# The high and low parts of w_a and w_b: taken apart by pieces in the attention stage instead of during the expert search

## The chip, the cores and the metric

One core of one Trainium2 chip. The metric is the device time of one execution in microseconds (us). Engines are named as in the profile: PE is TensorE (PEld its weight loads), DVE is VectorE, ACT is ScalarE, POOL is GpSimd, SP is SyncE; a "q" behind a name is that engine's queue, from which transfers are issued. The profile gives PE's granted clock as a share of 2.4 GHz: 1.00 is 2.4 GHz and 0.50 is 1.2 GHz.

## The reference, cut to what matters

```python
# attention: B, H, S, D = 4, 8, 768, 40
for t in range(S):
    m_new = maximum(f[t] + m, i[t])
    C = exp(f[t] + m - m_new) * C + exp(i[t] - m_new) * outer(v[t], k[t])
    n = exp(f[t] + m - m_new) * n + exp(i[t] - m_new) * k[t]
    y[t] = sigmoid(o[t]) * (C @ q[t]) / maximum(abs(n @ q[t]), 1)
# experts: 3072 tokens of 320, 8 experts, 384 tokens to each
logits = x @ w_gate
# the highest logits first: a token goes to an expert that has room
out[mask] = relu(x[mask] @ w1[e]) @ w2[e]          # F = 1024
# third layer, for every token
a = x @ w_a;  b = x @ w_b;  out = (a * b) @ w_out   # 320 -> 1536 -> 320
```

Everything is float32. The kernel multiplies in a shorter format (fp32r) and keeps the precision by splitting each matrix in two: the high part is the matrix rounded to fp32r, the low part is the matrix less its high part.

## The kernel before, in words

**Attention** (`attention`, from L85). The sequence is cut in C = 6 chunks of 128 steps; with B = 4 batches that makes 24 units, u = 4c + b. Each engine walks through the units in its own order, and they are tied by semaphores. The first and the last chunk are written out; the four between run in a hardware loop (`each`, L47).

- PE, per unit: psI from the state (L444), psC from wv (L452), the logits of unit u-2 (L418), psO (L461, after DVE's prob), then the scores psS of unit u+1 (L404), the exponents psE of unit u+2 (L395) and the transposes psT of unit u-1 (L412).
- ACT, per unit: the exponential of psE (L356), the issue of three transfers of q (L329), in the unit with b = 3 also the sigmoid of the gates with two table loads (L322, L363), then the store of y of unit u-2 (L343) and the copy xt of the transposes of unit u-2 (L348), for which it waits.
- POOL, per unit: st_old from the state (L286), wv of the next unit (L258), the mask of the next unit (L264, on the tile decay), and the new state (L271), for which it waits for DVE's L592.
- DVE, per unit: prob (L581), the normalization of the unit before (L559), num from psI (L586), the gated y of the unit before (L570), st_add from psC (L592; the profile calls its tile work), the logits' copy (L553), then, waiting for psO, **the sum of the values** num + psO (L598), denh (L600), den (L602) and the reciprocal (L605), on which the next normalization depends.
- SP issues the loads of qks and toks some four units ahead, after the scores and the psO of the unit whose buffers are refilled, and once a chunk the rows and the gates.

After its last unit POOL writes the whole numbers that the search needs into `ints` (L294 to L303).

**Search and experts** (`experts`, from L674). DVE and PE search for the first expert to be full in 11 rounds: DVE compares (cmp, L1133), PE counts (psT, L967 and L978), DVE narrows the range (L1191, with eq and key at L1195 and L1197 after some rounds). Then DVE picks the tokens (L1204 on) and places them (at_slot, L1270), POOL gathers them (L852), and PE starts on w1 and w2 of the first expert. The eight turns of the experts follow, each with the third layer (L929 to L952), which reads w_a and w_b as wa and wb: [128, 5, 1536], blocks 0 and 1 the high parts of rows 0 to 255, block 2 the high part of rows 256 to 319 in partitions 0 to 63 and its low part in partitions 64 to 127, blocks 3 and 4 the low parts of rows 0 to 255.

wa and wb are filled at the start of `experts`, beside the search: SP loads both matrices whole (L831 to L834), ACT copies the high parts (L1074 to L1076, two instructions of 128 x 4608), and POOL subtracts: L858, two instructions of 64 x 1536, and L863, eight of 128 x 768. POOL's gather (L852) stands behind them.

Of the kernel before, what the change touches and what calls it, by code (L numbers as in the profile page):

```python
# [16 lines left out]
P = 128  # L17
# [37 lines left out]
def build(nc, qk, tok, ig, fg, w_gate, w1, w2, w_a, w_b, w_out, out, xs, parts):  # L55
    with ExitStack() as ctx:
        logit = ctx.enter_context(nc.sbuf_tensor("logit", [P, TILES, E], F32))
        identf = ctx.enter_context(nc.sbuf_tensor("identf", [P, P], F32))

        wa = ctx.enter_context(nc.sbuf_tensor("wa", [P, 5, F2], F32R))  # L60
        wb = ctx.enter_context(nc.sbuf_tensor("wb", [P, 5, F2], F32R))
        second = (wa, wb)
        fixed = search_tensors(nc, ctx)
        with ExitStack() as inner:
            attention(nc, inner, logit, identf, qk, tok, ig, fg, w_gate, xs, parts, fixed)
        with ExitStack() as inner:
            experts(nc, inner, logit, identf, second, w_a, w_b, w_out, w1, w2, xs, out, fixed)
# [17 lines left out]
def attention(nc, ctx, logit, identf, qk, tok, ig, fg, w_gate, xs, parts, fixed):  # L85
# [53 lines left out]
    ints = sb("ints", [P, 384], I32)  # L139
# [21 lines left out]
    y_out1 y_out0 row_in parts_out diag_done st_scaled masked mrow_zero made cast_done reloaded""".split()  # L161
# [5 lines left out]
    block = ctx.enter_context(nc.Block())  # L167

# [4 lines left out]
    def _(sp):  # L173
# [3 lines left out]
        def load_gates(c):  # L177
            sp.dma_start(gate[:, bass.ds(c, 1), :, :].rearrange("p c b n -> p (c b) n"),
                         tok[bass.ds(c, 1), :, :, TOK:TOK + DM].rearrange("c b t n -> t (c b) n")).then_inc(sm["og_in"], 16)

# [9 lines left out]
        def chunk(c):  # L190
            for b in range(B):
# [20 lines left out]
                else:  # L212
                    sp.wait_ge(sm["o_ready"], u - B + 1)
                    sp.dma_start(toks[b][:, 0:TOK], tok[bass.ds(c, 1), b, :, 0:TOK].rearrange("c t n -> (c t) n")).then_inc(tok_in[b], 16)
                    if b == 1:
                        sp.wait_ge(sm["e_ready"], c * B)
                        load_rows(c)
            if not (isinstance(c, int) and c == C - 1):
                load_gates(c + 1)
        each(sp, C, chunk)  # L220

    @block.gpsimd
    def _(pool):
# [56 lines left out]
        for u in range(TILES):  # L280
# [12 lines left out]
            new_state(u)  # L293
        pool.iota(rowi, [[P, C], [S, B]], base=0, channel_multiplier=1).then_inc(sm["made"], 1)  # L294
# [18 lines left out]
    def _(act):  # L313
# [5 lines left out]
        def open_gates(c):  # L319
            act.wait_ge(sm["og_in"], 16 * (c + 1))  # L320
            g = gate[:, bass.ds(c, 1), :, :].rearrange("p c b n -> p (c b n)")
            act.activation(g, g, ACT.Sigmoid).then_inc(sm["gate_ready"], 1)  # L322

# [26 lines left out]
        def chunk(c):  # L350
            for b in range(B):
# [6 lines left out]
                if not (isinstance(c, int) and c == C - 1 and b):  # L358
                    load_turned(u + B - 1, (c + 1, b - 1) if b else (c, B - 1))
                if b == 3 and not (isinstance(c, int) and c == C - 1):  # L360
# [115 lines left out]
    def _(dve):  # L476
# [95 lines left out]

        def chunk(c):
            for b in range(B):
# [18 lines left out]
                if not (isinstance(c, int) and c == 0 and b < 2):  # L593
                    keep_logits(u - 2, (c, b - 2) if b > 1 else (c - 1, b + 2))

# [78 lines left out]
def experts(nc, ctx, logit, identf, second, w_a, w_b, w_out, w1, w2, xs, out, fixed):  # L674
# [24 lines left out]
    wab_in = ("wa_in", "wb_in")  # L699
# [5 lines left out]
    a_sb = [sb(f"a_sb{n}", [P, CAP]) for n in range(2)]  # L705
    ab = [sb(f"ab{n}", [P, CAP]) for n in range(2)]
# [15 lines left out]
    h_lo = [sb(f"h_lo{n}", [P, CAP], F32R) for n in range(2)]  # L722
    ab_hi = [sb(f"ab_hi{n}", [P, CAP], F32R) for n in range(2)]
# [74 lines left out]
    wa_in wb_in wab_hi wab_lo member_ready ranked x2_mm out_mm slots_ready slots_mm expert_known grouped parts_ready""".split()  # L798
# [17 lines left out]
    def _(sp):  # L816
# [30 lines left out]
    def _(pool):  # L847
# [31 lines left out]
    def _(pe):  # L879
# [49 lines left out]
        def pair(k, g, between_a=None, between_b=None):  # L929
            if isinstance(k, int) and k == 0 and g % GQ == 0:  # L930
                pe.wait_ge(sm["wab_lo"], 2 + 2 * (g // GQ + 1))
# [121 lines left out]
    def _(act):  # L1053
# [14 lines left out]
        def high_out(q):  # L1068
            act.wait_ge(wo_in[q % 2], 16 * (q // 2 + 1))
            if q == 0:  # L1070
                act.wait_ge(sm["wab_lo"], 2 + 2 * Q)
# [9 lines left out]
        def turn(k, beside):  # L1081
# [23 lines left out]
            for g in range(GT):  # L1105
                act.wait_ge(sm["ab_mm"], k * GT + g + 1)
                at_least(act, sm["ab_done"], k * GT + g - 1)
                if early and g == 0:
                    act.wait_ge(sm["wab_lo"], 2 + 2 * Q)
# [368 lines left out]
```

## Time and profile before

| | us |
|---|---|
| median of 3 runs | 939.88 (936.88 to 940.74) |
| the profiled execution | 947.86 |
| its span, first to last instruction | 946.1 |
| PE busy | 820.5 (87%) |
| DVE busy | 619.5 (65%) |
| ACT busy | 273.4 (29%) |
| POOL busy | 169.3 (18%) |
| attention | to about 163 |
| search, until PE starts on w1 | about 163 to 226 |
| eight turns of the experts | about 226 to 946 |

The profiled execution took 947.86 us, 1.7 us more than its span. Times in rows are counted from the start of the span. A row of the timeline has the start, the duration, engine, line, operation, the tile written and the tiles read, their shapes and the count; what stands in brackets is how long the engine had been idle before it and who ended that. Matmul rows of one group are merged.

### The profile page before, as it was taken

The page shows a single profiled execution, that of the slowest core. Times are in us where ns is not written, and L with a number is a line of the kernel's source. Part 1 is how long each engine was busy: PE and PEld are TensorE (multiplying, and loading weights), DVE is VectorE, ACT ScalarE, POOL GpSimd, SP SyncE. Part 2 cuts the span into 40 slices and gives each one's busy share as a digit, 9 for nine tenths or more (in the row PEclk, how much of TensorE's full clock was granted, in tenths as well). Part 3 has the DMA queues.
Part 4 walks back from the last instruction along what each step waited for, and adds up shares of the span by engine and source line. Part 5 has one row for each costly group of instructions (what it writes and reads, how often), then busy time and mean ns, then how long its engine had stood idle before and what let it go on. Part 6 is the DMA issues. An engine that isn't in the chain of part 4 may idle for free.

```text
span 946.1 us, 16640 instructions
## 1 busy us (share of the span) xinstructions
PE 820.5 (87%) x5858; PEld 757.7 (80%) x5858; DVE 619.5 (65%) x1644; ACT 273.4 (29%) x490; POOL 169.3 (18%) x195
## 2 busy tenths in 40 slices
PE   1999997314799899979997999899989989999995
PEld 1999997214689878978897889789878988998995
DVE  7688888576557865785677557755876683374222
ACT  4444441302223412331233123312422241233221
POOL 6665664261000110000011001100110011011001
PEclk9999999555789999999998999999999999999998
DMA  4766651612202200220031004100400120041000
GB/s 118 242 211 214 218 171 48 186 28 85 73 21 82 84 21 1 69 76 21 0 99 65 0 0 115 48 0 11 132 21 0 61 82 21 1 131 35 1 1 21
DMA packets 51620, 66.60 MB, mean 70 GB/s; under 512 B 6376, under 2 KB 42232, under 8 KB 51576
## 3 DMA queue, kind: packets, MB, share of 16 engines
q1 hardware_dynamic: 37352, 50.31, 17.5%
q0 software_dynamic: 2368, 7.88, 2.9%
q10 hardware_dynamic: 11856, 7.87, 2.7%
q8 instruction: 22, 0.36, 0.1%
q14 instruction: 22, 0.18, 0.1%
HBM read 57.88 MB, written 8.16 MB: 70 GB/s over the span
## 4 chain that ended last, share of the span: by engine, by line
PE 48%; DVE 23%; issue 5%; ACT 4%; DMA 2%; POOL 1%; ACTq 0%; DVEq 0%; POOLq 0%
PE psA L897 18%; PE acc L920 11%; PE psB L897 8%; PE acc L947 6%; DVE at_slot L1270 2%; DVE ab L1356 2%; DVE w_lo L1294 2%; DMA xg<-xs_dram,idx_g 2%; DVE cmp L1133 2%; ACT ab_hi L1103 2%; DVE w_lo L1290 2%; DVE ab_lo L1360 1%; DVE w_hi L1292 1%; PE psT L978 1%; DVE o_sb L1437 1%
## 5 line engine op out<-in xcount | busy, mean ns | idle before, releaser
L897 PE MATMUL psA<-x_hi,wa 128*128 128x384 f32 x480 | 136.1, 348 | 0.5 <-DVE x_lo L1382 0.4
L897 PE MATMUL psB<-x_hi,wb 128*128 128x384 f32 x480 | 131.8, 339 | 0.0
L852 POOL DMA_INDIRECT xg<-xs_dram,idx_g x24 | 24.9, 1036 | 466.8 <-DVE idx_g L1284 462.0
L1110 ACT COPY a_sb<-psA 128x384 f32<-128x384 f32 x96 | 46.1, 481 | 193.0 <-PE psB L897 193.0
L897 PE MATMUL psA<-x_lo,wa 128*128 128x384 f32 x288 | 96.8, 336 | 0.0
L897 PE MATMUL psB<-x_lo,wb 128*128 128x384 f32 x288 | 96.5, 335 | 0.0
L947 PE MATMUL acc<-wo_hi,ab_hi 128*128 128x320 f32 x288 | 92.1, 320 | 1.0 <-DVE ab_lo L1360 1.0
L1089 ACT ACTIVATE h_hi<-psA 128x384 fp32r<-128x384 f32 x64 | 31.5, 492 | 205.9 <-PE psA L897 197.9
L1356 DVE TENSOR_TENSOR ab<-a_sb,psB 128x384 f32<-128x384 f32 x96 | 53.0, 552 | 55.6 <-ACT a_sb L1110 55.2
L947 PE MATMUL acc<-wo_lo,ab_hi 128*128 128x320 f32 x288 | 88.8, 308 | 0.0
L947 PE MATMUL acc<-wo_hi,ab_lo 128*128 128x320 f32 x288 | 88.7, 308 | 0.0
L897 PE MATMUL psA<-x_hi,w_hi 128*128 128x384 f32 x192 | 76.5, 399 | 13.5 <-DVE w_lo L1297 7.5
L1360 DVE TENSOR_TENSOR ab_lo<-ab,ab_hi 128x384 fp32r<-128x384 f32 x96 | 53.6, 559 | 52.2 <-ACT ab_hi L1103 48.2
L897 PEld LDWEIGHTS psA<-x_hi,wa 128*128 128x128 f32 x480 | 83.1, 188 | 4.1 <-DVE x_lo L1382 2.1
L897 PEld LDWEIGHTS psB<-x_hi,wb 128*128 128x128 f32 x480 | 86.0, 188 | 0.1
L920 PE MATMUL acc<-h_hi,w_hi 128*128 128x384 f32 x192 | 73.0, 380 | 14.5 <-DVE h_lo L1349 14.5
L1103 ACT CAST ab_hi<-ab 128x384 fp32r<-128x384 f32 x96 | 49.2, 513 | 82.7 <-DVE ab L1356 80.3
L897 PE MATMUL psA<-x_lo,w_hi 128*128 128x384 f32 x192 | 67.9, 354 | 0.0
L920 PE MATMUL acc<-h_lo,w_hi 128*128 128x384 f32 x192 | 67.3, 350 | 0.0
L920 PE MATMUL acc<-h_hi,w_lo 128*128 128x384 f32 x192 | 67.2, 350 | 0.0
L874 POOL DMA_INDIRECT out_dram<-o_sb,idx_s x24 | 23.7, 986 | 219.9 <-DVE o_sb L1437 215.0
L947 PEld LDWEIGHTS acc<-wo_hi,ab_hi 128*128 128x128 f32 x288 | 54.1, 188 | 2.1 <-DVE ab_lo L1360 1.2
(236 smaller groups left out, 1744.7 us busy)
## 6 DMA issues: line engine op xcount, KB each, us to landing
w_raw<-in_w_dram SPq DMA_DIRECT2D x32, 320.0 KB, 3.3
w_raw<-in_w_dram SPq DMA_DIRECT2D x32, 256.0 KB, 3.0
toks<-in_tok_dram SPq DMA_DIRECT2D x24, 324.0 KB, 3.5
qks<-in_qk_dram SPq DMA_DIRECT2D x48, 160.0 KB
w_raw<-in_w_dram SPq DMA_DIRECT2D x64, 64.0 KB, 2.8
gate<-in_tok_dram SPq DMA_DIRECT2D x6, 640.0 KB, 5.4
xs_dram<-y ACTq DMA_DIRECT2D x24, 160.0 KB, 3.2
qst<-in_qk_dram ACTq DMA_DIRECT2D x48, 60.0 KB
```

Of the source, the lines that this page charges most:

```text
L852: pool.indirect_dma_start(out=xg[:, t, 0:DM], out_offset=None, in_=xrows, in_offset=bass.IndirectOffsetOnAxis(ap=idx_g[:, t:t + 1], axis=0 ...
L874: pool.indirect_dma_start(out=out, out_offset=bass.IndirectOffsetOnAxis(ap=idx_s[:, t:t + 1], axis=0), in_=o_sb[:, t, :], in_offset=None). ...
L897: last = pe.matmul(ps, w, x, start=(n == 0), stop=(n == len(steps) - 1))
L920: last = pe.matmul(acc[m][:, 0:CAP], w[q][:, f % FQ, c], x[n][:, :], start=(f == 0 and j == 0), stop=(f == FT - 1 and j == 2))
L947: last = pe.matmul(acc[t][:, 0:DM], x[n][:, c], w[:, g, :], start=(g == 0 and j == 0), stop=(g == GT - 1 and j == 2))
L1089: act.activation(h_hi[f % 2][:, :], psA[f % 2][:, 0:CAP], ACT.Relu).then_inc(sm["h_hi_ready"], 1)
L1103: act.copy(ab_hi[g % 2][:, :], ab[g % 2][:, :]).then_inc(sm["ab_hi_ready"], 1)
L1110: act.copy(a_sb[g % 2][:, :], psA[g % 2][:, 0:CAP]).then_inc(sm["a_copied"], 1)
L1133: dve.scalar_tensor_tensor(out=cmp[:, :, :], in0=key[lv][:, :].unsqueeze(2).broadcast_to([P, TILES, 16]), scalar=start_at[:, lv:lv + 1] if ...
L1270: dve.tensor_tensor(at_slot[i][:, :, :], prow[:, i * ST:(i + 1) * ST].unsqueeze(2).broadcast_to([P, ST, P]), slot[:, :].unsqueeze(1).broad ...
L1356: dve.tensor_tensor(ab[g % 2][:, :], a_sb[g % 2][:, :], psB[g % 2][:, 0:CAP], ALU.mult).then_inc(sm["ab_done"], 1)
L1360: dve.tensor_tensor(ab_lo[g % 2][:, :], ab[g % 2][:, :], f32(ab_hi[g % 2][:, :]), ALU.subtract).then_inc(sm["ab_ready"], 1)
```

## The change

SP, in the attention stage, loads w_a and w_b in six pieces of 256 columns each (`load_piece`, three transfers, 384 KB together), two units or more ahead of their use. ACT copies the high part of a piece of w_a in the units with b = 0 and of a piece of w_b in those with b = 2, behind its exponential and its issues (`split_high`, 128 x 768). DVE subtracts half a piece in every unit, between the logits' copy and the sum of the values (`split_low`): two instructions, 128 x 256 and 64 x 128 (partitions 64 to 127). `ints` now lies in the piece's buffer, so POOL waits for the last subtraction before it writes there. In `experts` the loads, the two copies, POOL's ten subtractions and the waits for them are gone.

```diff
+    piece = sb("piece", [P, 2, 3, F2 // C])
+    ints = piece[:, 0, :, :].rearrange("p k f -> p (k f)").bitcast(I32)
+    FB = F2 // C
...
+        def load_piece(c, i):
+            at_least(sp, sm[f"piece_lo{i}"], 4 * c)
+            w, cols = (w_a, w_b)[i], bass.ds(c * FB, FB)
+            sp.dma_start(piece[:, i, 0:2, :], w[0:2 * P, cols].rearrange("(k p) f -> p k f", p=P)).then_inc(sm[f"piece_in{i}"], 16)
+            sp.dma_start(piece[0:64, i, 2, :], w[2 * P:DM, cols]).then_inc(sm[f"piece_in{i}"], 16)
+            sp.dma_start(piece[64:P, i, 2, :], w[2 * P:DM, cols]).then_inc(sm[f"piece_in{i}"], 16)
...
                     if b == 1:
                         sp.wait_ge(sm["e_ready"], c * B)
                         load_rows(c)
+                    if b == 0:
+                        load_piece(c - 1, 1)
+                if b == 2:
+                    load_piece(c, 0)
...
         each(sp, C, chunk)
+        load_piece(C - 1, 1)
...
             new_state(u)
+        for i in range(2):
+            pool.wait_ge(sm[f"piece_lo{i}"], 4 * C)
...
+        def split_high(c, i):
+            act.wait_ge(sm[f"piece_in{i}"], 48 * (c + 1))
+            act.copy(second[i][:, 0:3, bass.ds(c * FB, FB)], piece[:, i, :, :]).then_inc(sm[f"piece_hi{i}"], 1)
...
                     load_turned(u + B - 1, (c + 1, b - 1) if b else (c, B - 1))
+                if b % 2 == 0:
+                    split_high(c, b // 2)
...
+        def split_low(c, b):
+            i = b // 2
+            w, at = second[i], b % 2 * (FB // 2)
+            part, cols = slice(at, at + FB // 2), bass.ds(c * FB + at, FB // 2)
+            dve.wait_ge(sm[f"piece_hi{i}"], c + 1)
+            dve.tensor_tensor(w[:, 3:5, cols], piece[:, i, 0:2, part], w[:, 0:2, cols].bitcast(F32), ALU.subtract).then_inc(sm[f"piece_lo{i}"], 1)
+            dve.tensor_tensor(w[64:P, 2, cols], piece[64:P, i, 2, part], w[64:P, 2, cols].bitcast(F32), ALU.subtract).then_inc(sm[f"piece_lo{i}"], 1)
...
                     keep_logits(u - 2, (c, b - 2) if b > 1 else (c - 1, b + 2))
+                split_low(c, b)
 
                 dve.wait_ge(sm["o_ready"], u + 1)
...
-    with nc.sbuf_tensor("wab_raw", [P, 2, 3, F2], F32) as wab_raw:
-        pass
...
-        for i, w in enumerate((w_a, w_b)):
-            sp.dma_start(wab_raw[:, i, 0:2, :], w[0:2 * P, :].rearrange("(k p) f -> p k f", p=P)).then_inc(sm[wab_in[i]], 16)
-            sp.dma_start(wab_raw[0:64, i, 2, :], w[2 * P:DM, :]).then_inc(sm[wab_in[i]], 16)
-            sp.dma_start(wab_raw[64:P, i, 2, :], w[2 * P:DM, :]).then_inc(sm[wab_in[i]], 16)
...
-        for i in range(2):
-            pool.wait_ge(sm["wab_hi"], i + 1)
-            pool.tensor_tensor(second[i][64:P, 2, :], wab_raw[64:P, i, 2, :], f32(second[i][64:P, 2, :]), ALU.subtract).then_inc(sm["wab_lo"], 1)
-        pool.wait_ge(sm["wab_lo"], 2)
-        for q in range(Q):
-            cols_ = slice(q * GQ * P, (q + 1) * GQ * P)
-            for i in range(2):
-                pool.tensor_tensor(second[i][:, 3:5, cols_], wab_raw[:, i, 0:2, cols_], f32(second[i][:, 0:2, cols_]), ALU.subtract
-                                   ).then_inc(sm["wab_lo"], 1)
-        pool.wait_ge(sm["wab_lo"], 2 + 2 * Q)
...
-        for i in range(2):
-            act.wait_ge(sm[wab_in[i]], 48)
-            act.copy(second[i][:, 0:3, :], wab_raw[:, i, :, :]).then_inc(sm["wab_hi"], 1)
```

The buffers a_sb and ab are declared further down, with the same sizes.

## Rows read from the trace of the kernel before

**Rows 1.** Stretches view: length, busy us and count by engine, clock, DMA share, GB/s.

```profile
20.00:163.00 143.00, 140.01 (x1478) 133.53 (x1478) 120.32 (x268) 53.73 (x69) 84.14 (x107) 1.00 0.59 184
```

**Rows 2.** Timeline, PE: the second and the last score products.

```profile
31.30 1.16 PE L404 MATMUL psS<-qks 40*128 40x128 f32 x16
...
152.57 1.16 PE L404 MATMUL psS<-qks 40*128 40x128 f32 x16
```

**Rows 3.** Timeline, DVE: one unit and the next one's start.

```profile
126.58 1.23 DVE L581 TENSOR_TENSOR prob<-psS,decay 128x1024 f32<-128x1024 f32 x1
...
128.53 1.06 DVE L570 TENSOR_TENSOR y<-work,gate 128x320 f32<-128x320 f32 x1
129.51 0.49 DVE L592 TENSOR_TENSOR work<-psC,diag 120x328 f32<-120x328 f32 x1
...
130.41 0.50 DVE L598 TENSOR_TENSOR num<-num,psO 128x328 f32<-128x328 f32 x1 [0.34 <-PE psO L461]
130.95 0.17 DVE L600 TENSOR_SCALAR denh<-num 128x8 f32<-128x8 f32 x1
131.15 0.61 DVE L602 SCALAR_TENSOR_TENSOR den<-num,denh 128x8 f32<-128x8 f32 x1
...
131.99 1.22 DVE L581 TENSOR_TENSOR prob<-psS,decay 128x1024 f32<-128x1024 f32 x1
...
133.94 0.48 DVE L570 TENSOR_TENSOR y<-work,gate 128x320 f32<-128x320 f32 x1
```

**Rows 4.** Timeline, POOL: the same unit.

```profile
128.16 1.09 POOL L264 TENSOR_SCALAR_AFFINE_SELECT decay<-decay 128x1024 f32<-128x1024 f32 x1 [1.13 <-ACT decay L356]
130.15 0.89 POOL L271 TENSOR_TENSOR state<-st_old,work 120x328 f32<-120x328 f32 x1 [0.90 <-DVE work L592]
130.99 0.74 POOL L286 TENSOR_TENSOR st_old<-state,dec 120x328 f32<-120x328 f32 x1
131.68 0.74 POOL L258 TENSOR_TENSOR wv<-toks,gw 128x328 f32<-128x328 f32 x1
```

**Rows 5.** Waits view, 60 to 150 us (us in total, times, longest).

```profile
ACT xt L348 <- PE psT L412: 51.6, 13, 4.1
```

**Rows 6.** Chain of waits, search stage (start us, us, what).

```profile
169.09 0.63 DVE cmp L1133
...
175.66 0.26 DVE eq L1195
...
178.41 3.77 DVE cmp L1133
...
188.12 1.76 DVE eq L1195
...
195.45 2.27 DVE cmp L1133
...
203.12 1.89 DVE sel L1204
```

**Rows 7.** Timeline, POOL: the first low part.

```profile
178.34 3.42 POOL L858 TENSOR_TENSOR wa<-wab_raw,wa 64x1536 fp32r<-64x1536 f32 x1 [18.52 <-ACT wa L1076]
```

**Rows 8.** Timeline, ACT and DVE: the same operations on other weights.

```profile
213.55 0.83 ACT L1064 CAST w_hi<-w_raw 128x768 fp32r<-128x768 f32 x1 [27.62 <-DMA w_raw<-in_w_dram]
...
215.98 0.42 DVE L1292 TENSOR_TENSOR w_hi<-w_raw,w_hi 64x256 fp32r<-64x256 f32 x1
...
217.29 0.29 DVE L1297 TENSOR_TENSOR w_lo<-w_raw,w_hi 128x128 fp32r<-128x128 f32 x1
```

**Rows 9.** Timeline, ACT, SP and DVE: the first units.

```profile
25.72 1.02 ACT L356 ACTIVATE decay<-psE 128x1024 f32<-128x1024 f32 x1 [1.22 <-PE psE L395]
...
25.91 0.48 SPq L211 DMA_DIRECT2D toks<-in_tok_dram  x1
...
32.58 1.23 DVE L581 TENSOR_TENSOR prob<-psS,decay 128x1024 f32<-128x1024 f32 x1
```

**Rows 10.** DMA issues of the attention stage (KB each, median us to landing).

```profile
toks<-in_tok_dram SPq DMA_DIRECT2D x22, 324.0 KB, 3.5
```

More of the change, by code:

```diff
@@ L64, in build @@
         with ExitStack() as inner:
-            attention(nc, inner, logit, identf, qk, tok, ig, fg, w_gate, xs, parts, fixed)
+            attention(nc, inner, logit, identf, second, w_a, w_b, qk, tok, ig, fg, w_gate, xs, parts, fixed)
         with ExitStack() as inner:
-            experts(nc, inner, logit, identf, second, w_a, w_b, w_out, w1, w2, xs, out, fixed)
+            experts(nc, inner, logit, identf, second, w_out, w1, w2, xs, out, fixed)
 def search_tensors(nc, ctx):
@@ L82, in search_tensors, with attention @@
     }
-def attention(nc, ctx, logit, identf, qk, tok, ig, fg, w_gate, xs, parts, fixed):
+def attention(nc, ctx, logit, identf, second, w_a, w_b, qk, tok, ig, fg, w_gate, xs, parts, fixed):
     def sb(name, shape, dt=F32):
@@ L137, in attention @@
     scaled = work[0][:, 0:DM]
-    ints = sb("ints", [P, 384], I32)
+    piece = sb("piece", [P, 2, 3, F2 // C])
+    ints = piece[:, 0, :, :].rearrange("p k f -> p (k f)").bitcast(I32)
     rowi, tilei, pi, digiti = ints[:, 0:24], ints[:, 24:48], ints[:, 48:49], ints[:, 64:80]
@@ L160, in attention @@
     state_done i_used o_used den_half den_done r_done scale_done y_ready og_in gate_ready wv_ready wg_zero y_zero
-    y_out1 y_out0 row_in parts_out diag_done st_scaled masked mrow_zero made cast_done reloaded""".split()
+    y_out1 y_out0 row_in parts_out piece_in0 piece_in1 piece_hi0 piece_hi1 piece_lo0 piece_lo1 diag_done st_scaled masked mrow_zero made cast_done reloaded""".split()
     sm = {n: sem(n) for n in names}
@@ L671, with experts @@
 GI = GJ * 16
-def experts(nc, ctx, logit, identf, second, w_a, w_b, w_out, w1, w2, xs, out, fixed):
+def experts(nc, ctx, logit, identf, second, w_out, w1, w2, xs, out, fixed):
     def sb(name, shape, dt=F32):
@@ L698, in experts @@
     wa, wb = second
-    wab_in = ("wa_in", "wb_in")
-    with nc.sbuf_tensor("wab_raw", [P, 2, 3, F2], F32) as wab_raw:
-        pass
     wo_hi = sb("wo_hi", [P, GT, DM], F32R)
     wo_lo = sb("wo_lo", [P, GT, DM], F32R)
-    a_sb = [sb(f"a_sb{n}", [P, CAP]) for n in range(2)]
-    ab = [sb(f"ab{n}", [P, CAP]) for n in range(2)]
     w1_raw = [sb(f"w1_raw{n}", [P, 3, FQ * P]) for n in range(2)]
@@ L722, in experts @@
     h_lo = [sb(f"h_lo{n}", [P, CAP], F32R) for n in range(2)]
+    a_sb = [sb(f"a_sb{n}", [P, CAP]) for n in range(2)]
+    ab = [sb(f"ab{n}", [P, CAP]) for n in range(2)]
     ab_hi = [sb(f"ab_hi{n}", [P, CAP], F32R) for n in range(2)]
@@ L797, in experts @@
     wo_hi_done wo_split made counted spread given_ready given_sum v_step cmp_ready full_ready
-    wa_in wb_in wab_hi wab_lo member_ready ranked x2_mm out_mm slots_ready slots_mm expert_known grouped parts_ready""".split()
+    member_ready ranked x2_mm out_mm slots_ready slots_mm expert_known grouped parts_ready""".split()
     sm = {n: sem(n) for n in names}
@@ L929, in pair @@
         def pair(k, g, between_a=None, between_b=None):
-            if isinstance(k, int) and k == 0 and g % GQ == 0:
-                pe.wait_ge(sm["wab_lo"], 2 + 2 * (g // GQ + 1))
             at_least(pe, sm["ab_done"], k * GT + g - 1)
@@ L1069, in high_out @@
             act.wait_ge(wo_in[q % 2], 16 * (q // 2 + 1))
-            if q == 0:
-                act.wait_ge(sm["wab_lo"], 2 + 2 * Q)
             act.copy(wo_hi[:, q * GQ:(q + 1) * GQ, :], wo_raw[q % 2]).then_inc(sm["wo_hi_done"], 1)
-        for i in range(2):
-            act.wait_ge(sm[wab_in[i]], 48)
-            act.copy(second[i][:, 0:3, :], wab_raw[:, i, :, :]).then_inc(sm["wab_hi"], 1)
         high_parts(0, 0)
@@ L1107, in turn @@
                 at_least(act, sm["ab_done"], k * GT + g - 1)
-                if early and g == 0:
-                    act.wait_ge(sm["wab_lo"], 2 + 2 * Q)
                 act.copy(a_sb[g % 2][:, :], psA[g % 2][:, 0:CAP]).then_inc(sm["a_copied"], 1)
```

## The prediction, made before the changed kernel ran

> **What bounds the kernel now.** I read the stretches first, then the timelines of PE, DVE and POOL over one unit, the waits, and last the chain of waits through the search. In attention PE is busy 140 of 143 us at the full clock [rows 1]: it runs without a gap, and its score products start at 31.30 for unit 1 and 152.57 for unit 23 [rows 2], so a unit takes 121.27 / 22 = 5.51 us. DVE is close behind. The unit shown goes from prob at 126.58 to prob at 131.99, 5.41 us, and DVE idles only 0.34 of it, in front of the sum of the values [rows 3]. DVE is also held up by POOL. The gated y takes 1.06 us while POOL's mask runs and 0.48 one unit later without it; it ends 0.34 after the mask, the time of its 320 columns. den has 8 columns, takes 0.61, and ends 0.03 after POOL's st_old [rows 3, 4]. So a DVE instruction with two SBUF inputs waits out a POOL instruction. The sum of the values and prob, which read PSUM, keep their 0.50 and 1.22. In the search the same happens with longer partners: cmp takes 0.63, but 3.77 beside POOL's low part of 3.42, which began just before it [rows 6, 7]. These cmp lie on the chain.
>
> **What goes: the search.** Seven DVE instructions are stretched by POOL's ten subtractions: cmp 3.77; eq 1.76 and its like behind it, key, 1.85; three cmp of 2.11, 2.27 and 2.27; sel 1.89. Together 15.92. Undisturbed they are four cmp of 0.63, two of 0.26 as eq, and sel about 0.17 as denh in rows 3: 3.21. Gain 12.7 us, all on the chain [rows 3, 6]. ACT's two copies, the six loads and POOL's waits there are covered by the search and give nothing more: the gather waits for the token list anyway.
>
> **What comes: DVE.** The 128 x 256 instruction costs what 64 x 256 does, 0.42, the 64 x 128 one what 128 x 128 does, 0.29 [rows 8]. Both have two SBUF inputs, and they stand just where POOL starts its three instructions state, st_old, wv. So I lay the unit out from the end of st_add, 130.00 (129.51 + 0.49), with a waiting instruction taken in turn:
> - State first (it starts 0.15 after st_add; the logits' copy and the loop's address work may delay DVE that long). State ends 131.04, the first subtraction 0.28 later (256 columns against 320 in 0.34), 131.32. st_old takes 0.69 (spacing 130.99 to 131.68), to 132.01; the second subtraction, 132.15; wv 0.70, 132.85. The sum of the values runs 132.18 to 132.68, denh then waits for wv, 132.88, and den (0.20 with its gap), reciprocal (0.23) bring prob to 133.31. It was 131.99: 3.31 us after st_add, not 1.99.
> - Subtraction first: it ends 130.49, state about 131.30, the second subtraction 131.44, st_old 132.14, wv 132.84, den 132.87, prob 133.10: 3.10 after st_add.
>
> On the other side of the unit, the mask comes earlier against DVE, as it is timed by PE through the exponential. y then goes back from 1.06 to 0.48 and the normalization, which ends 1.6 after prob, is held by some 0.12: prob to the end of st_add goes from 3.42 to 2.96. The unit becomes 6.06 to 6.27, middle 6.17, against PE's 5.51. Between the two orders I take the middle, since neither row decides a difference of some hundredths. 22 units x 0.66 = 14.5 us. PE's work of a unit still fits: it has idle time in front of psO instead.
>
> By the Trainium skill ("SBUF — State Buffer", section "Who interferes with whom") VectorE and GpSimd share an exclusive lock: a VectorE instruction with two SBUF inputs and a GpSimd instruction that reads SBUF block one another in full, in order of issue. It speaks against this change, and its order of issue would give 3.10 or 3.31 as above; the stretched y, den and cmp agree with it, while without such a lock the sum is that of the first rival.
>
> **ACT and SP.** The high part is 0.83 for 128 x 768 [rows 8], in every second unit, where ACT waits about 4 us in front of xt [rows 5]: nothing, if the piece has arrived. Piece 0 of a chunk is issued two units before its copy is due in DVE, but ACT comes to it right behind an early exponential. With three issues of about 0.5 each and 3.5 us to landing as for toks [rows 9, 10], it lands 5 us after the psO that releases the load, and the copy ends about when xt becomes ready. If that cover is gone, xt, the logits and the next exponential move. I take 1 us for all chunk borders, bounds 0 and 5. SP's own queue has room: about 2.5 us of issues in a unit of 5.5, and qks behind the piece moves by 1.5 us, more than a unit ahead of need. POOL's wait at the end finds the subtractions done; the last unit's fall into an idle stretch of DVE.
>
> **The start.** The first piece can't be ahead. SP issues it behind toks of 25.91, so from 26.4 to about 28, and it lands near 31.5 [rows 9, 10]. ACT copies to 32.4, and only then comes the exponential that ran at 25.72; its mask adds 1.1, and prob of unit 1 starts at about 34.6 rather than 32.58: 2.0 us. Bounds 0.5 (landing at 30) and 4 (a crowded start).
>
> **The sum.** -12.7 + 14.5 + 1.0 + 2.0 = +4.8 us. Against the profiled execution of 947.9 that is 952.7; the median of the runs shown is 8 us lower, and as the terms are differences within one execution I put them on that median: 939.9 + 4.8 = 944.7. A difference of 0.5%, 4.7 us, is about what a measurement of this kernel can tell from no change.
>
> **The rivals.**
> 1. Faster: the subtractions cost DVE only their own time. In place they take about 0.75 us (0.42 + 0.29, and starts that no longer overlap); a unit without DVE's wait is 5.41 - 0.34 = 5.07, so 5.82 against 5.51, 0.31 x 22 = 6.8. With 3.0 for start and borders: 939.9 - 12.7 + 9.8 = 937.0. If y is no longer held up, PE stays the bound and it is 930.2. It decides if the unit stays below 5.51 + 9.7 / 22 = 5.95. For it: in many units y loses half a microsecond to the mask that it could win back. Against: den would have to get in front of wv, and it comes 0.7 us too late. Centre 934.
> 2. POOL never yields: both subtractions wait for all three of its instructions. They end at 132.97 and prob comes at 134.13, a unit of 7.1: 22 x 1.6 = 35, 965. Against: denh at 130.95 runs in 0.17 between state and st_old [rows 3, 4].
> 3. The pieces come late in each chunk, 2 us for each of five, on top of the main case: 954. For it: twelve pieces of 384 KB add 4.6 MB to some 26 MB (184 GB/s for 143 us), with the DMA share at 0.59 already [rows 1].
> 4. The search's stretches are not POOL's doing, so nothing is gained: 957. Rows 6 and 7 speak plainly against it.
>
> TensorE: the stage before runs at 2.4 GHz with PE busy throughout [rows 1]. The gaps of 0.7 us that I expect in each unit leave it busy nine tenths of the time, and I cost them at nothing more.
>
> **Chances.** The main case 0.52; its own range is 22 units of 0.44 to 0.86, start 0.5 to 4 and borders 0 to 5, mostly 938 to 953. Rival 1 0.28, rival 2 0.05, rival 3 0.12, rival 4 0.03. Faster than 935.2: 0.20 of rival 1 and 0.04 of the main case, 0.24. Within: 0.08 and 0.20, 0.28. Slower than 944.6: 0.28 and the other three, 0.48. The range 931 to 956 leaves out rivals 2 and 4 and the tail of rival 1, and takes in rival 3.
>
> **What would show it.** In the changed profile the cmp of the search are all 0.63, and from the first cmp to at_slot it is 12 to 13 us shorter. The psS of units 1 and 23 are 135 to 137 us apart, not 121; PE idles in front of psO, waiting for prob; the two subtractions take 0.4 to 1.3 us with POOL's state or st_old ending just before them, and den ends just after wv. prob of unit 1 starts at 34 to 35. ACT's xt has an idle time in front of it in the units with b = 0. The prediction is wrong if psS keeps a distance below 5.95 a unit, or if the experts' turns, which nothing here touches, change by several microseconds.

## The result, and the profile after

The changed kernel takes 948.43 us (median of 4 runs, 947.51 to 950.06), the kernel before beside it 940.31 (936.88 to 941.27): a ratio of 1.0086, 95% interval 1.0054 to 1.0119, so 5 to 11 us slower. The prediction said +4.8 us on 939.9, 944.7, with a range of 931 to 956.

The stages say more than the sum, and they must, since the profiled run of before (947.86) was slower than the runs beside it, at a mean clock of 0.944 over the span against 0.955 in the profile of after. I read the end of attention from best, the first reduction of the search, and the end of the search from the first at_slot:

| us from the start of the span | before | after | difference |
|---|---|---|---|
| prob of unit 1 | 32.58 | 35.86 | +3.3 |
| prob of unit 23 | 154.16 | 175.31 | +21.2 |
| best (attention is over) | 162.94 | 185.53 | +22.6 |
| at_slot (search is over) | 211.00 | 220.98 | +10.0 |
| end of the span | 946.1 | 945.8 | -0.3 |

The change costs 22.6 us in attention and gives back 12.6 in the search, +10.0 by then. The rest of the span is 735.1 us before and 724.8 after, though nothing in it was changed; in the profiles of the twelve experiments below it lies between 723 and 731. So it is the profile of before that stands out, and -0.3 between the two spans says nothing of the change; +10.0 by stages is what the medians (+8.1, interval 5 to 11) agree with. The stretches view of after, attention stage (length, busy us and count of PE, PEld, DVE, ACT, POOL, clock, DMA share, GB/s):

```profile
20.00:185.00 165.00, 148.55 (x1478) 138.31 (x1478) 146.81 (x314) 64.19 (x81) 86.41 (x107) 0.96 0.62 188
```

Against [rows 1] the same 1478 matmuls of attention leave PE idle 16 us, and their clock is no longer 1.00. DVE has gone from 120 busy us to 147 and is the bound.

The chain of waits of after, search stage, answers to [rows 6]:

```profile
189.49 0.63 DVE cmp L1142
...
198.27 0.25 DVE eq L1204
...
214.73 0.25 DVE sel L1213
...
220.98 3.57 DVE at_slot L1279 x4
```

No cmp is stretched any more, and eq and sel take 0.25.

One unit of DVE, timeline of after, for [rows 3]:

```profile
126.13 1.22 DVE L616 TENSOR_TENSOR prob<-psS,decay 128x1024 f32<-128x1024 f32 x1
127.27 1.10 DVE L586 TENSOR_TENSOR work<-num,rden 128x320 f32<-128x320 f32 x1
...
128.71 0.47 DVE L597 TENSOR_TENSOR y<-work,gate 128x320 f32<-128x320 f32 x1
129.11 0.48 DVE L627 TENSOR_TENSOR work<-psC,diag 120x328 f32<-120x328 f32 x1
...
129.59 0.41 DVE L605 TENSOR_TENSOR wb<-piece,wb 128x256 f32 x1
130.03 0.85 DVE L606 TENSOR_TENSOR wb<-piece,wb 64x128 f32 x1
...
131.45 0.76 DVE L636 TENSOR_SCALAR denh<-num 128x8 f32<-128x8 f32 x1
132.24 0.17 DVE L638 SCALAR_TENSOR_TENSOR den<-num,denh 128x8 f32<-128x8 f32 x1
...
133.09 1.23 DVE L616 TENSOR_TENSOR prob<-psS,decay 128x1024 f32<-128x1024 f32 x1 [0.44 <-issue]
```

POOL in the same unit, timeline of after, for [rows 4]:

```profile
126.94 1.09 POOL L282 TENSOR_SCALAR_AFFINE_SELECT decay<-decay 128x1024 f32<-128x1024 f32 x1 [1.27 <-ACT decay L381]
129.74 0.99 POOL L289 TENSOR_TENSOR state<-st_old,work 120x328 f32<-120x328 f32 x1 [1.71 <-DVE work L627]
130.70 0.78 POOL L304 TENSOR_TENSOR st_old<-state,dec 120x328 f32<-120x328 f32 x1
131.44 0.73 POOL L276 TENSOR_TENSOR wv<-toks,gw 128x328 f32<-128x328 f32 x1
```

Read the two together. The first subtraction gets in front of state. The second is issued while state runs (until 130.73) and ends at 130.88, 0.15 after it: 0.85 us for 128 columns that take 0.29 where nothing holds them. denh, 8 columns, is issued 0.01 after wv, and ends at 132.21, 0.04 after wv. On the other side the mask, which used to hold y, now runs from 126.94, before the normalization at 127.27, and holds that one until 0.34 after its own end. The groups of DVE from 50 to 150 us show how regular that is (count | busy us, mean ns | idle). Before:

```profile
L570 DVE TENSOR_TENSOR y<-work,gate 128x320 f32<-128x320 f32 x18 | 15.7, 870 | 0.0
L602 DVE SCALAR_TENSOR_TENSOR den<-num,denh 128x8 f32<-128x8 f32 x18 | 11.5, 641 | 0.6
L559 DVE TENSOR_TENSOR work<-num,rden 128x320 f32<-128x320 f32 x19 | 9.2, 482 | 0.0
```

After:

```profile
L636 DVE TENSOR_SCALAR denh<-num 128x8 f32<-128x8 f32 x16 | 12.1, 757 | 0.5
L586 DVE TENSOR_TENSOR work<-num,rden 128x320 f32<-128x320 f32 x16 | 11.8, 737 | 0.0
L597 DVE TENSOR_TENSOR y<-work,gate 128x320 f32<-128x320 f32 x16 | 8.5, 532 | 0.0
L606 DVE TENSOR_TENSOR wa<-piece,wa 64x128 f32 x8 | 6.9, 866 | 0.2
```

On average y wins 0.34 and the normalization loses 0.26. The wait that den had is now denh's.

The start, ACT's and SP's timeline of after, for [rows 9]:

```profile
24.24 0.43 SPq L189 DMA_DIRECT2D piece<-in_w_a_dram  x1
...
31.92 0.83 ACT L347 CAST wa<-piece 128x768 fp32r<-128x768 f32 x1 [7.43 <-DMA piece<-in_w_a_dram]
...
32.65 1.02 ACT L381 ACTIVATE decay<-psE 128x1024 f32<-128x1024 f32 x1
...
40.97 0.83 ACT L347 CAST wb<-piece 128x768 fp32r<-128x768 f32 x1 [5.69 <-DMA piece<-in_w_b_dram]
```

Twice ACT stands in front of a piece that has not landed. Behind the first piece stands the exponential that ran at 25.72 in before, behind the second the copy xt and the next exponential. The small transfers of the first piece need 5.9 us to land (DMA issues of after, 20 to 30 us):

```profile
piece<-in_w_a_dram SPq DMA_DIRECT2D x2, 64.0 KB, 5.9
```

The waits view of after, 20 to 185 us (us in total, times, longest), has both waits and what PE pays:

```profile
ACT wa L347 <- DMA piece<-in_w_a_dram: 18.4, 6, 7.4
...
ACT wb L347 <- DMA piece<-in_w_b_dram: 14.2, 5, 5.7
PE psO L488 <- DVE prob L616: 10.3, 15, 1.3
```

And right there PE loses its clock, stretches view of after:

```profile
35.00:45.00 10.00, 8.87 (x56) 8.15 (x55) 8.08 (x15) 1.97 (x4) 5.76 (x7) 0.52 0.60 188
```

In before the clock is 1.00 from 30 to 50 us (1.00 is 2.4 GHz, 0.50 is 1.2 GHz).

### The profile page after: what moved, and what is told of

Read it like the earlier page. It is cut to its first block, busy times and chain, and to the rows that moved or that the text cites. A ratio compares the mean times of both kernels' runs of the same rounds, so it can differ in the third digit from the quotient of the medians.

```text
span 945.8 us, 16800 instructions
## 1 busy us (share of the span) xinstructions
PE 819.5 (87%) x5858; PEld 754.8 (80%) x5858; DVE 633.6 (67%) x1692; ACT 275.6 (29%) x500; POOL 149.4 (16%) x185
## 4 chain that ended last, share of the span: by engine, by line
PE 48%; DVE 22%; issue 4%; ACT 4%; DMA 1%; POOL 1%; ACTq 0%; DVEq 0%
PE psA L915 18%; PE acc L938 11%; PE psB L915 9%; PE acc L963 6%; DVE w_lo L1303 2%; DVE ab L1365 2%; DVE at_slot L1279 2%; DVE w_lo L1299 2%; DVE ab_lo L1369 2%; ACT ab_hi L1114 2%; DVE cmp L1142 1%; DVE w_hi L1301 1%; PE psT L994 1%; DMA xg<-xs_dram,idx_g 1%; DVE o_sb L1446 1%
## 5 line engine op out<-in xcount | busy, mean ns | idle before, releaser
L915 PE MATMUL psA<-x_hi,w_hi 128*128 128x384 f32 x192 | 74.6, 389 | 13.6 <-DVE w_lo L1306 7.5
L938 PE MATMUL acc<-h_hi,w_hi 128*128 128x384 f32 x192 | 70.7, 368 | 14.6 <-DVE h_lo L1358 14.6
L938 PE MATMUL acc<-h_lo,w_hi 128*128 128x384 f32 x192 | 65.2, 339 | 0.0
L938 PE MATMUL acc<-h_hi,w_lo 128*128 128x384 f32 x192 | 65.1, 339 | 0.0
L488 PE MATMUL psO<-toks,prob 128*128 128x96 f32 x384 | 50.1, 285 | 10.8 <-DVE prob L616 10.3
```

Source lines behind the costliest of these rows:

```text
L488: last = pe.matmul(psO[:, h * DA:h * DA + NP_], prob[n][:, h, :], toks[b][:, H * D + h * DA:H * D + h * DA + NP_], start=True, stop=True)
L915: last = pe.matmul(ps, w, x, start=(n == 0), stop=(n == len(steps) - 1))
L938: last = pe.matmul(acc[m][:, 0:CAP], w[q][:, f % FQ, c], x[n][:, :], start=(f == 0 and j == 0), stop=(f == FT - 1 and j == 2))
```

## The experiments

Twelve kernels ran. All times are medians, with the kernel before in the same series beside them: 941.37 for the first four, 939.73 for the next four, 941.12 for three, 939.53 for the last.

### The search alone, and the attention stage without the subtractions

First the gain by itself: the kernel before, with POOL's ten subtractions left out of the search. Two copies by ACT put the high parts where the low parts belong, so this kernel leaves the low parts out.

```diff
-            pool.tensor_tensor(second[i][64:P, 2, :], wab_raw[64:P, i, 2, :], f32(second[i][64:P, 2, :]), ALU.subtract).then_inc(sm["wab_lo"], 1)
...
-                pool.tensor_tensor(second[i][:, 3:5, cols_], wab_raw[:, i, 0:2, cols_], f32(second[i][:, 0:2, cols_]), ALU.subtract
-                                   ).then_inc(sm["wab_lo"], 1)
```

> The kernel before without POOL's ten subtractions beside the search (the low parts of w_a and w_b are filled by two ACT copies of the high ones instead, so the third layer's numbers are not the reference's). Theory (a DVE instruction with two SBUF inputs waits out a POOL instruction): the seven stretched instructions are gone, the way from the first reduction of the search (best) to at_slot falls from 48.1 to 35.4 us, and the time from 940.3 to 927.6. Rival (the stretches come from the loads or ACT's copies, or the time goes elsewhere): the way stays at 48, the time at 940.

Measured: 925.92 us (923.77 to 926.65), ratio 0.9829 [0.9785, 0.9874]. From best to at_slot 162.62 to 198.07, 35.45 us, exactly as long as in the changed kernel, against 48.06 before. So the search's gain is POOL's doing, 12.6 us, and it is not given back later. The median fell by 15.4, with an interval of 4 us either way that takes in the 12.6.

Then the attention stage with everything of the change but DVE's two instructions, and with the loads earlier than the change has them (the low parts left out as above; SP and POOL, which waited for the subtractions before they reused a piece, now wait for ACT's copy):

```diff
                     if b == 0:
+                        load_piece(0, 0)
+                        load_piece(0, 1)
                         sp.wait_ge(sm["a3_ready"], 3)
...
                         load_rows(c)
-                    if b == 0:
-                        load_piece(c - 1, 1)
-                if b == 2:
-                    load_piece(c, 0)
+                        load_piece(c, 0)
+                    if b == 3:
+                        load_piece(c, 1)
...
-        load_piece(C - 1, 1)
...
-            dve.tensor_tensor(w[:, 3:5, cols], piece[:, i, 0:2, part], w[:, 0:2, cols].bitcast(F32), ALU.subtract).then_inc(sm[f"piece_lo{i}"], 1)
-            dve.tensor_tensor(w[64:P, 2, cols], piece[64:P, i, 2, part], w[64:P, 2, cols].bitcast(F32), ALU.subtract).then_inc(sm[f"piece_lo{i}"], 1)
```

> The changed kernel without DVE's subtractions, with the first pieces loaded in SP's idle time before unit 0 and the later ones a unit earlier (the low parts' blocks are filled by two ACT copies beside the search, so the third layer's numbers are not the reference's). Theory (DVE's subtractions make the units longer): prob to prob is back at 5.5 us a unit, prob of unit 1 at 32.6, and with the shorter search the time is 927 to 929. Rival (ACT's copies and the pieces' transfers cost time of their own in attention): units of 5.7 or more, 932 or more.

Measured: 927.43 us (923.72 to 930.78), ratio 0.9865 [0.9814, 0.9916]. Units of 5.57 us from prob to prob (5.53 before), best at 162.91 (before 162.94). Twelve loads of 384 KB, SP's issues for them and ACT's twelve copies cost attention nothing, if the pieces come in time. What is left of the 22.6 us is DVE's instructions and the moment of the loads, and the next run tells them apart.

### The loads' moment

The changed kernel with the same early loads, and its subtractions in place: the diff above without its last three lines.

> The changed kernel with the loads moved only: the first pieces before unit 0, in SP's idle time, the later ones a unit earlier. Theory (the first piece's landing delays ACT's second exponential by 3.3 us, PE's idle time there costs it its full clock for 10 us, some 4 us more): prob of unit 1 back at 32.6, the first three units 16 to 19 us together instead of 24.5, clock 1.00 throughout, the time 941. Rival (the low clock there is chance, the start is hidden): 948, and the low clock again.

Measured: 941.66 us (940.27 to 947.73, 10 runs), ratio 1.0028 [0.9996, 1.0061]; prob of unit 1 at 32.54, clock 1.00 from 20 to 80 us, best at 178.81. The moment of the loads is worth 6.7 us of the 22.6, and DVE's two instructions the other 15.9 (178.81 less 162.91). In the medians of the two series the loads are worth 6.8, by the two ratios to the kernel before 5.5, with about 4 us either way. Two kernels split it. In the first, only the load of w_a's first piece is early:

```diff
                     if b == 0:
+                        load_piece(0, 0)
                         sp.wait_ge(sm["a3_ready"], 3)
...
-                if b == 2:
+                if b == 2 and not (isinstance(c, int) and c == 0):
                     load_piece(c, 0)
```

> The changed kernel with one edit: the load of the first chunk's piece of w_a alone stands in front of the wait for the a rows; every other load stays where the change has it, the piece of w_b at the first unit of the next chunk. With all loads early the time was 941.66 against 948.43 of the change. Theory: all of that comes from this one load. It lets the exponential of unit 1 run at its old time (3.3 us at prob of unit 1), and PE, which then idles less in the first units, keeps its full clock (2.7 us in units 2 to 4). Prob of unit 1 starts at 32.5 to 32.8, the granted clock stays at 1.00 from 30 to 50 us, prob of unit 23 comes at 169 to 170, and the run takes 941.5 to 943. Rival: the w_b copy that waited 5.7 us in unit 3 causes the low clock by itself. Then prob of unit 1 is early, but units 2 to 4 stay at 7 us and more with the clock at 0.5 for a while, and the run takes 944 to 946.

Measured: 949.18 us (945.57 to 954.05, 11 runs), ratio 1.0083 [1.0053, 1.0112]. Neither time came: nothing was won, although prob of unit 1 is early (31.87). The rest is what the rival described, units 2 to 4 long and the clock low. ACT's timeline and the DMA issues (30 to 45 us) of this kernel say why:

```profile
25.70 1.02 ACT L382 ACTIVATE decay<-psE 128x1024 f32<-128x1024 f32 x1
...
40.62 0.83 ACT L348 CAST wb<-piece 128x768 fp32r<-128x768 f32 x1 [8.05 <-DMA piece<-in_w_b_dram]
```

```profile
piece<-in_w_b_dram SPq DMA_DIRECT2D x2, 64.0 KB, 7.1
```

The exponential that the copy of w_a's piece held up is on time again (25.70). But ACT then runs on to the copy of w_b's piece and waits there 8.05 us for transfers of 64 KB that need 7.1 us to land, against 3.1 as the median over the stage in the changed kernel. Stretches of this kernel:

```profile
30.00:35.00 5.00, 4.90 (x54) 4.47 (x53) 4.87 (x10) 1.02 (x1) 2.58 (x4) 1.00 0.98 328
35.00:40.00 5.00, 3.24 (x41) 2.87 (x39) 4.83 (x10) 0.00 (x0) 2.36 (x3) 1.00 0.75 236
...
45.00:50.00 5.00, 5.00 (x37) 4.57 (x37) 2.12 (x6) 1.82 (x3) 1.37 (x2) 0.50 0.38 120
```

The fourth number of busy time is ACT's: it does nothing from 35 to 40. PE then idles 3.64 us for xt (to 41.88), and at 45 to 50 its clock is 0.50. DMA is at 0.98 of its time when the piece is issued. In the second kernel the pieces of w_b alone are early:

```diff
                     if b == 0:
+                        load_piece(0, 1)
                         sp.wait_ge(sm["a3_ready"], 3)
...
-                    if b == 0:
-                        load_piece(c - 1, 1)
+                    if b == 3:
+                        load_piece(c, 1)
...
-        load_piece(C - 1, 1)
```

> The other half: only the pieces of w_b are loaded early (the first in front of the wait for the a rows, the others one unit earlier than in the change), the pieces of w_a stay where the change has them. Both halves early gave 941.66, neither 948.43, w_a's first alone 949.18 against a kernel before of 941.12: with it ACT still waited 8.05 us for the first piece of w_b, whose transfers of 64 KB took 7.1 us to land at 30 to 40 us. Theory: each of the two late landings costs its wait and the low clock that follows, and they overlap when both are there. Here the first piece of w_a alone is late: prob of unit 1 at 35.5 to 36, 3.3 us behind, no wait of ACT for w_b, the clock at 0.5 for less than the 10 us of the change, prob of unit 23 at 172 to 173.5, and the run takes 944.5 to 946.5. Rival: the loss comes from the pieces of w_b alone, and the late first exponential is caught up: prob of unit 23 at 169 to 170 and 941 to 943.

Measured: 948.86 us (946.00 to 954.27, 6 runs), ratio 1.0096 [1.0058, 1.0134]. The trace does what the theory says, up to the clock. Timeline of ACT and a stretch of this kernel:

```profile
32.05 0.83 ACT L347 CAST wa<-piece 128x768 fp32r<-128x768 f32 x1 [7.54 <-DMA piece<-in_w_a_dram]
...
36.39 0.83 ACT L347 CAST wb<-piece 128x768 fp32r<-128x768 f32 x1 [0.98 <-issue]
```

```profile
35.00:40.00 5.00, 3.60 (x38) 3.32 (x39) 4.91 (x9) 1.24 (x2) 4.10 (x5) 1.00 0.61 203
```

| | prob 1 | prob 23 | best | time |
|---|---|---|---|---|
| all as in the change | 35.86 | 175.31 | 185.53 | 948.43 |
| w_a's first piece early | 31.87 | 175.15 | 185.42 | 949.18 |
| w_b's pieces early | 36.01 | 172.69 | 182.60 | 948.86 |
| all early | 32.54 | 169.23 | 178.81 | 941.66 |

Each of the two late landings costs by itself: w_a's 3.5 us (172.69 less 169.23), w_b's 5.9 (175.15 less 169.23), the two together 6.1. After a late piece of w_a ACT reaches w_b's later and waits 5.69 us there and not 8.05, so part of the second wait is already paid. Of the clock the theory was wrong: with w_a's piece late alone it did not fall at all. And the profiled execution of this kernel, 946.0, was the lowest of its six; the 2.6 us that its trace shows against the change are not in its median. An interval of 3.6 us either way can't decide that. So the split of the start rests on one trace each, and for the total only the pair "all early" against the change is shown.

### DVE's own time or its waits

Two reductions over the same columns in place of the subtractions, with one input from SBUF (loads early; low parts left out as above):

```diff
-            dve.tensor_tensor(w[:, 3:5, cols], piece[:, i, 0:2, part], w[:, 0:2, cols].bitcast(F32), ALU.subtract).then_inc(sm[f"piece_lo{i}"], 1)
-            dve.tensor_tensor(w[64:P, 2, cols], piece[64:P, i, 2, part], w[64:P, 2, cols].bitcast(F32), ALU.subtract).then_inc(sm[f"piece_lo{i}"], 1)
+            dve.tensor_reduce(peak[:, b % 2, :], piece[:, i, 0:2, part], AX.X, ALU.max).then_inc(sm[f"piece_lo{i}"], 1)
+            dve.tensor_reduce(peak2[64:P, b % 2, 0:1], piece[64:P, i, 2:3, part], AX.X, ALU.max).then_inc(sm[f"piece_lo{i}"], 1)
```

> As the run with early loads, but each subtraction is a maximum over the same columns of the piece: the same time on DVE, one SBUF input instead of two (the low parts' blocks are filled by ACT copies of the high ones beside the search, so the third layer's numbers are not the reference's). Theory (the lock with POOL makes the larger part of the cost): neither instruction is stretched, state starts and ends on time, but the sum of the values is still 0.75 us later and den still misses its place in front of wv, so from st_add's end to prob 2.7 us instead of 3.05, units of 5.8 to 6.0, time about 935. Rival (only DVE's own time counts): the unit is as long as with the subtractions, 6.3, and the time within 2 us of the run with early loads alone.

Measured: 935.10 us (932.23 to 941.11, 10 runs), ratio 0.9942 [0.9912, 0.9972], 6.6 below the early loads with subtractions. The timeline of DVE of this kernel:

```profile
126.43 0.41 DVE L607 TENSOR_REDUCE peak<-piece 128x2 f32<-128x256 f32 x1
126.87 0.28 DVE L608 TENSOR_REDUCE peak<-piece 64x1 f32<-64x128 f32 x1
...
127.72 0.48 DVE L638 TENSOR_SCALAR denh<-num 128x8 f32<-128x8 f32 x1
128.23 0.65 DVE L640 SCALAR_TENSOR_TENSOR den<-num,denh 128x8 f32<-128x8 f32 x1
```

The second instruction takes 0.28 here and 0.85 as a subtraction, although POOL's state starts just before it in both (126.59). By the Trainium skill ("SBUF — State Buffer", section "Who interferes with whom") a reduction never contends with GpSimd, and a two-input instruction does; the pair 0.28 and 0.85 agrees. Units are 6.00 us instead of 6.21: Two instructions that wait for nothing make 0.43 of the 0.64 between 5.57 and 6.21, and the second one's wait behind state only 0.21, since den and the normalization are then held longer (0.65, and 1.34 to 1.42 in most second units).

### The order against POOL

With early loads, POOL's mask in front of its wv:

```diff
+                mask(u + 1)
                 weigh(u + 1)
-                mask(u + 1)
```

> As the run with early loads, and POOL makes the next unit's mask before its wv. Theory (den waits for wv, which POOL starts just in front of it): denh and den take 0.2 us each again, from st_add's end to prob 2.3 us instead of 3.05; wv then falls on the normalization or y and gives a part back, so units of 5.8 to 6.0 instead of 6.21, 934 to 938 against 941.7. Rival (DVE's own 0.75 us is what counts): 6.2 and 941 to 942.

Measured: 936.01 us (933.63 to 940.97, 10 runs), ratio 0.9955 [0.9931, 0.9979]. Units of 5.98. DVE's timeline of this kernel:

```profile
126.73 0.88 DVE L606 TENSOR_TENSOR wa<-piece,wa 64x128 f32 x1
...
128.17 0.17 DVE L636 TENSOR_SCALAR denh<-num 128x8 f32<-128x8 f32 x1
128.37 0.17 DVE L638 SCALAR_TENSOR_TENSOR den<-num,denh 128x8 f32<-128x8 f32 x1
```

With wv gone from there, denh and den take 0.17 each and the unit is 0.23 shorter than with early loads alone, while the second subtraction still waits out state. Next, the subtractions in front of st_add, before POOL may start state (POOL as in the change):

```diff
+                split_low(c, b)
                 dve.wait_ge(sm["cs_ready"], u + 1)
...
                     keep_logits(u - 2, (c, b - 2) if b > 1 else (c - 1, b + 2))
-                split_low(c, b)
```

> As the run with early loads, with DVE's two subtractions in front of st_add instead of in front of the sum of the values. Theory: there POOL has finished its mask, so both run in 0.42 and 0.29 us; state, st_old and wv start 0.75 later, but den is behind st_old only, 2.0 us after st_add's end instead of 3.05; prob to st_add's end grows from 3.2 to about 3.95. Units of 5.8 to 6.1, 934 to 939 against 941.7. Rival (the place in DVE's order does not matter): 6.2 and 941 to 942.

Measured: 938.09 us (935.23 to 946.02, 10 runs), ratio 1.000 [0.997, 1.003]. Units of 6.10. DVE's timeline of this kernel:

```profile
120.84 0.41 DVE L605 TENSOR_TENSOR wb<-piece,wb 128x256 f32 x1
121.29 0.29 DVE L606 TENSOR_TENSOR wb<-piece,wb 64x128 f32 x1
...
122.62 0.55 DVE L636 TENSOR_SCALAR denh<-num 128x8 f32<-128x8 f32 x1
123.20 0.65 DVE L638 SCALAR_TENSOR_TENSOR den<-num,denh 128x8 f32<-128x8 f32 x1
```

Both subtractions run at their own 0.41 and 0.29. But of the 0.56 us won there only 0.11 reach the unit, since state, now later, holds denh, and st_old holds den.

### The subtractions on POOL

With early loads, POOL subtracts half a piece in each unit, first between wv and the mask, then behind the mask and in front of the state. DVE is left as it was.

Between wv and the mask (`split_low` is now POOL's and holds the same two `tensor_tensor`):

```diff
                 weigh(u + 1)
+            split_low(u)
+            if u + 1 < TILES:
                 mask(u + 1)
...
-                split_low(c, b)
```

Behind the mask:

```diff
                 weigh(u + 1)
                 mask(u + 1)
+            split_low(u)
...
-                split_low(c, b)
```

> Early loads, and the subtractions made by POOL in each unit between wv and the mask, none by DVE. Theory: POOL idles there about 1.1 us while DVE is in prob, which reads PSUM and isn't held up; POOL's two instructions take 0.6 and 0.35, so the unit stays at PE's 5.5 to 5.6, the search is 12.6 us shorter, and the time is 928 to 930, faster than both kernels. Rival (more work on POOL holds up the normalization, y or the mask in any place): units of 5.8 or more, 935 or more.

Measured: 929.91 us (928.18 to 932.32), ratio 0.9896 [0.9854, 0.9937].

> The same two instructions on POOL, but behind the mask, in front of the new state. Theory (what counts is which instruction of the other engine is under way): they meet the normalization and y, which are held for up to 1 us more, and may push state; units of 5.8 to 6.2, 935 to 941. Rival (POOL has 2 us idle a unit and any place will do): as with them between wv and the mask, within 1 us.

Measured: 927.52 us (923.88 to 929.17), ratio 0.9852 [0.9808, 0.9895]. The theory fell: the place that should have cost 5 to 11 us more was no slower. Both ran again, side by side.

> The kernel with POOL's subtractions between wv and the mask once more, in more rounds, beside the one with them behind the mask. Theory of place: a late mask costs, a late state costs nothing, so this one is slower than the other by 1.5 to 3 us, 929 to 930.5. Rival: the two places are equal, both within 1 us of 928.5.

> The kernel with POOL's subtractions behind the mask and in front of the state once more, in more rounds. Theory of place: 927 to 928, 1.5 to 3 us below the one with the subtractions in front of the mask. Rival: equal to it within 1 us.

Measured: 929.94 us (927.26 to 932.72, 6 runs) and 928.17 (926.09 to 934.39, 6 runs), ratios 0.9856 [0.9816, 0.9897] and 0.9861 [0.9816, 0.9907]. In the traces at_slot starts at 200.3 and 199.6. With intervals of about 4 us either way neither expectation is decided: the order behind the mask was 2.4 and 1.8 us lower in two series, and 1.1 and 0.7 earlier at the start of at_slot. POOL's and DVE's timeline, behind the mask, second series:

```profile
117.89 1.09 POOL L282 TENSOR_SCALAR_AFFINE_SELECT decay<-decay 128x1024 f32<-128x1024 f32 x1 [0.28 <-ACT decay L393]
118.95 0.96 POOL L291 TENSOR_TENSOR wa<-piece,wa 128x256 fp32r<-128x256 f32 x1
119.98 0.46 POOL L293 TENSOR_TENSOR wa<-piece,wa 64x128 fp32r<-64x128 f32 x1
120.52 0.88 POOL L300 TENSOR_TENSOR state<-st_old,work 120x328 f32<-120x328 f32 x1
...
120.60 0.82 DVE L639 TENSOR_SCALAR denh<-num 128x8 f32<-128x8 f32 x1
121.46 0.65 DVE L641 SCALAR_TENSOR_TENSOR den<-num,denh 128x8 f32<-128x8 f32 x1
```

The subtractions fill the time in which POOL waited for st_add (0.90 in [rows 4]), and state follows at 120.52 for a st_add that ended at 119.74, 0.8 late. DVE pays for that: denh waits out state (0.82) and den st_old (0.65). But PE stays the bound (busy 124.3 of the 125 us from 30 to 155), so what one unit loses the next ones win back. Units are 5.63 us on average and both orders beat the kernel before by 10 to 13 us and the change by 18 to 21, while they compute all that it does.

## Why the prediction was right in sign and too low in size

By its own steps, against the stages:

| step | predicted | measured |
|---|---|---|
| the search | -12.7 | -12.6 |
| 22 units | +14.5 | +15.1 (all loads early) |
| borders of chunks | +1.0 | 0 |
| the start | +2.0 | +6.1 |
| after prob of unit 23 | 0 | +1.4 |
| sum | +4.8 | +10.0 by stages, +8.1 in the medians |

**The search** was right, term and cause: every cmp takes 0.63, and leaving out POOL's work alone gives the same 35.45 us.

**The unit** was right in its mechanism, and its number is in part luck. From the end of st_add to the next prob 3.10 was laid out with the subtraction first, and the rows show 3.05 in most units, with 0.44 more at the loop's edge in one of four. From prob to the end of st_add 2.96 was laid out, and it is 3.14 on average in the kernel with early loads. So the order that came was priced at 6.06 and took 6.21; the forecast, 6.17, is nearer only because it is the middle between this order and one that did not come. That DVE would be the bound and PE would idle in front of psO is in the waits (10.3 us). Two details were off: denh waits for wv, not den, at the same end, which costs nothing; and the normalization was said to be held by 0.12, but is held by 0.26 on average (0.54 to 0.67 in every second unit). The psS of units 1 and 23 stand 143 us apart (30.23 and 173.31), not 135 to 137, because the start's loss falls between them.

**The start is the term that was mis-sized.** The step reads "lands near 31.5 ... prob of unit 1 starts at about 34.6": the piece landed at 31.9, after it ACT took its copy and then the exponential, and prob came at 35.86: 3.3 us where 2.0 stood. That the landing came so near is luck: the step has SP issue the piece from 26.4 on and gives it 3.5 us; SP issued it from 24.24 on, and its small transfers took 5.9, two errors of about 2 us that cancel. What was missing is w_b's first piece. I gave all borders one microsecond with the landing time of the whole stage, 3.5 us; this one is issued while DMA is full, and its small transfers take 7 us. With its wait of 5.69 us and PE's low clock from 35 to 45 us, the stretch from prob of unit 1 to prob of unit 4 lost another 2.8. Together that is 6.1, beyond the upper bound of 4. "I cost them at nothing more" of the clock held in the steady units (1.00 from 50 us on, with gaps of up to 1.3) and failed in the start, behind 2.43 us of idle time. How much of the 2.8 is clock and how much is wait was not taken apart and stays open.

**The borders** after the first cost nothing: from prob of unit 4 on the units of the change and of the kernel with early loads are the same within 0.1. That ACT's waits there fall in time that it would spend waiting for xt is likely, but no run shows it.

**The end**: the last unit was said to hide its subtractions. It took 1.4 us more between prob of unit 23 and best. With early loads it is 0.8, the subtractions' time on DVE's chain; the other 0.6 is open.

**The rivals.** Rival 1, DVE's own time only, fell: it needed units below 5.95 us; the change has 6.21 with early loads, and even the kernel with the reductions has 6.00. Its price was 5.82; two instructions without a wait of their own still add 0.43 to 5.57, since den and the normalization keep their waits. Rival 2 fell, since both subtractions get a turn. Rival 3 was right in kind for one piece, and wrong in "each chunk". Rival 4 fell with the search.

One sign that the prediction named against itself did appear: from at_slot on, where nothing was changed, the two profiles differ by 10 us (735.1 and 724.8). As told above it is the profile of before that stands out; no run shows why beyond its lower clock.

One thing that the prediction didn't ask was what the 15.1 us buy. The same subtractions on POOL cost attention 1 to 3 us instead (best at 164 to 166, not 162.94).

## What to carry to other kernels

When work moves to an engine that is nearly the bound, write out one unit with the other engine's instructions beside it; that gave each half of the unit here to within 0.2 us. Then look where the gap is: POOL waited some 2 us in each unit (1.13 and 0.90 in [rows 4]) and DVE a third of a microsecond, so the instructions belong to POOL; both places that were tried there gave 928 to 930 us. And price a first load apart from the steady ones: with DMA full at the start the same 64 KB took 7 us instead of 3, and a copy in the middle of ACT's queue passed that on to everything behind it.

## What the runs showed of the hardware

- A wait moves to the next eligible instruction. Taking the 0.56 us wait off the second subtraction (0.85 to 0.29) shortened the unit by 0.11 only; taking wv away from denh (0.76 to 0.17) shortened it by 0.23.
- An instruction of 8 columns (denh, 0.17 alone) waits as fully as one of 320: 0.76 behind wv. denh has a single tensor input, and still it waited. By the Trainium skill ("SBUF — State Buffer", section "Who interferes with whom") a tensor_scalar whose operands meet the conditions can run in a mode that takes both port pairs, and so contends too. The 0.76 agrees; that denh runs in this mode no trace shows. The reduction's 0.28 beside state is the other side of the same rule.
- The 64x128 subtraction takes POOL 0.45 to 0.74 us and the 128x256 one 0.72 to 0.97, against 0.29 and 0.41 on DVE where nothing holds it.
- TensorE's granted clock fell to 0.50 in the start of the changed kernel, behind 2.43 us of idle time that ended at 33.81: it was 1.00 still from 34 to 35 us, with PE at work, 0.65 from 35 to 36 and 0.50 from 36 to 37. In the kernel with w_a's first piece early it fell behind 3.64 us. With w_b's pieces early it stayed at 1.00 behind 1.98 and 1.40 us. In before it is 1.00 from 20 to 163 us.
- Unchanged work of some 725 us, from at_slot to the end, moved by up to 12 us between single profiled executions (735.1 at a mean clock of 0.944 over the span, 723.3 at 0.963): more than the whole effect. Only stages and medians could be compared.
